# Three of four MLP GEMMs as seven block products, and each MLP over all tokens in turn

## The reference

```python
def _attn_ref(q, k, v, tau):                     # q, k, v: 1 x 6016 x 256
    qn = q / (np.linalg.norm(q, axis=1, keepdims=True) + 1e-06)
    kn = k / (np.linalg.norm(k, axis=1, keepdims=True) + 1e-06)
    s = kn.transpose(0, 2, 1) @ qn / tau         # 256 x 256
    s = s - s.max(-1, keepdims=True)
    a = np.exp(s)
    a /= a.sum(-1, keepdims=True) + 1e-09
    return v @ a

x = _attn_ref(q, k, v, tau).reshape(6016, 256)
h = x @ moe_w_in                                 # 256 x 2048
x = (h * np.cos(h)) @ moe_w_out                  # 2048 x 256
h = x @ moe2_w_in
y = (h * (1.0 / (1.0 + np.exp(-h)))) @ moe2_w_out
```

## Time and profile before

| | us |
|---|---|
| median of 3 executions (1125.02 to 1125.83) | 1125.22 |
| the profiled execution, span from first to last instruction | 1123.1 |
| PE busy in it | 1108.1 |
| ACT busy | 578.9 |
| DVE busy | 551.9 |
| POOL busy | 0.8 |
| first fold matmul starts | 60.07 |
| last matmul starts | 1119.57 |

### The profile page before, as it was taken

The page is one execution under the profiler, slowest core; times in us unless marked ns, Lnnn a source line. Parts: engine busy times, 40 slices in busy tenths (PEclk is TensorE's granted clock), DMA queues, the critical chain, the costliest instruction groups (busy, mean ns, idle before and its releaser), DMA issues.

```text
span 1123.1 us, 12484 instructions
## 1 busy us (share of the span) xinstructions
PE 1108.1 (99%) x4952; PEld 917.3 (82%) x4952; DVE 551.9 (49%) x505; ACT 578.9 (52%) x604; POOL 0.8 (0%) x7
## 2 busy tenths in 40 slices
PE   7999999999999999999999999999999999999998
PEld 7978788888888888888888888888888888889888
DVE  8879852562462463364265255256246346326312
ACT  7777753554554454355455455355455445446443
POOL 0000000000000000000000000000000000000000
PEclk9989999999999999999999999999999999999999
DMA  8823000000000000000000000000000000000000
GB/s 286 285 95 96 36 1 19 20 1 19 19 0 19 0 19 19 0 19 0 19 19 0 19 19 0 19 19 0 19 19 0 14 0 19 0 1 20 1 19 15
DMA packets 15539, 33.31 MB, mean 30 GB/s; under 512 B 1184, under 2 KB 5792, under 8 KB 15520
## 3 DMA queue, kind: packets, MB, share of 16 engines
q1 hardware_dynamic: 15520, 33.03, 8.7%
HBM read 26.87 MB, written 6.16 MB: 29 GB/s over the span
## 4 chain that ended last, share of the span: by engine, by line
PE 98%; DVE 1%; DMA 0%; ACT 0%; issue 0%; DVEq 0%
PE h_ps L638 16%; PE h_ps L639 16%; PE h_ps L637 16%; PE x_ps L637 8%; PE x_ps L638 8%; PE x_ps L639 8%; PE y_ps L638 8%; PE y_ps L637 8%; PE y_ps L639 8%; PE x_ps L652 2%; PE h_ps L654 1%; PE h_ps L656 1%; DMA qk_raw<-qk 0%; DVE qk_lo L457 0%; DVE work L510 0%; DVE work L517 0%
## 5 line engine op out<-in xcount | busy, mean ns | idle before, releaser
L498 DVE TENSOR_TENSOR g_lo<-work,g_hi 128x1024 fp32r<-128x1024 f32 (+1 forms) x192 | 230.4, 1200 | 285.1 <-ACT g_hi L378 273.0
L510 DVE SCALAR_TENSOR_TENSOR work<-work,h_ps 128x1024 f32<-128x1024 int32 (+1 forms) x96 | 115.1, 1199 | 156.4 <-ACT work L361 156.3
L361 ACT ACTIVATE work<-h_ps 128x1024 int32<-128x1024 f32 (+1 forms) x96 | 96.9, 1010 | 167.3 <-PE h_ps L639 167.2
L378 ACT ACTIVATE g_hi<-h_ps 128x1024 fp32r<-128x1024 f32 (+1 forms) x96 | 96.8, 1008 | 160.0 <-PE y_ps L639 124.7
L376 ACT ACTIVATE work<-h_ps 128x1024 f32<-128x1024 f32 (+1 forms) x96 | 96.8, 1008 | 135.8 <-PE h_ps L639 135.8
L637 PE MATMUL x_ps<-g_hi,w1out_hi 128*128 128x512 f32 (+1 forms) x384 | 150.0, 391 | 0.4 <-DVE x_lo L484 0.4
L638 PE MATMUL h_ps<-v_lo,wu_hi 128*128 128x512 f32 (+1 forms) x384 | 149.8, 390 | 0.0
L639 PE MATMUL h_ps<-v_hi,wu_lo 128*128 128x512 f32 (+1 forms) x384 | 149.8, 390 | 0.0
L638 PE MATMUL x_ps<-g_lo,w1out_hi 128*128 128x512 f32 (+1 forms) x384 | 149.8, 390 | 0.0
L637 PE MATMUL h_ps<-v_hi,wu_hi 128*128 128x512 f32 (+1 forms) x384 | 149.5, 389 | 0.0
L639 PE MATMUL x_ps<-g_hi,w1out_lo 128*128 128x512 f32 (+1 forms) x384 | 149.2, 389 | 0.0
(11 more groups left out here) (111 smaller groups left out, 1151.4 us busy)
## 6 DMA issues: line engine op xcount, KB each, us to landing
qk_raw<-qk SPq DMA_DIRECT2D x23, 512.0 KB, 4.7
v_raw<-vT SPq DMA_DIRECT2D x11, 512.0 KB, 3.8
yT<-y_out SPq DMA_DIRECT2D x11, 512.0 KB, 2.8
w_raw<-w_in SPq DMA_DIRECT2D x8, 512.0 KB, 5.4
w_raw<-w_out SPq DMA_DIRECT2D x8, 512.0 KB, 4.0
v_raw<-vT SPq DMA_DIRECT2D x1, 384.0 KB, 3.3
yT<-y_out SPq DMA_DIRECT2D x2, 192.0 KB, 1.9
qk_raw<-qk SPq DMA_DIRECT2D x1, 256.0 KB, 4.6
```

Source lines behind the costliest of these rows:

```text
L361: nc.scalar.activation(work_int[:, slot, :, 0:n], h, ACT.Identity, bias=0.25).then_inc(turns_ready, 1)
L378: nc.scalar.activation(g_hi[:, slot, :, 0:n], h, ACT.Silu).then_inc(g_hi_ready, 1)
L498: nc.vector.tensor_tensor(g_lo[:, slot, :, 0:n], work[:, slot, :, 0:n], g_hi[:, slot, :, 0:n], ALU.subtract).then_inc(g_ready, 1)
L510: nc.vector.scalar_tensor_tensor(out=work[:, slot, :, 0:n], in0=work_int[:, slot, :, 0:n], scalar=0.25, in1=h, op0=ALU.subtract, op1=ALU.s ...
```

## The change

Each step now takes a 2 x 2 block matrix of weights (two halves of the depth by two pairs of hidden blocks) with a 2 x 2 block of activations (two halves of the depth by two halves of a tile's tokens). In place of eight block products it forms seven, with sums and differences of the blocks as operands (the Winograd form of Strassen's scheme): `hidden(i, q)` is product i of step q. This is done for the first GEMM of both MLPs and the second of MLP 2. The second GEMM of MLP 1 stays as it is, in eight groups (`output1`).

- **Tiles.** Twelve tiles of 500 or 504 tokens, in two halves of 250 or 252, so that all MLP matmuls have 250 or 252 columns in place of 512. A tile has four steps of four hidden blocks.
- **Order.** MLP 1 runs over all tiles (steps 0 to 47), then MLP 2 (steps 48 to 95). x is stored to DRAM by tile and loaded again as MLP 2's input. All loops over steps are unrolled.
- **PSUM.** Products 1, 6, 7 and 4 accumulate one after the other in the same bank (two banks alternate by step), and ACT copies the sum out behind 1, 6 and 7 (`s1`, `s2`, `s3` into `s_part`). DVE adds products 2, 5 and 3 from banks 2 and 3 to these copies (`c11`, `c22`, `c12` into `h`). The fourth block stays in its bank.
- **Forms.** The activations' eight forms are made per tile from a DMA-loaded tile: three POOL ops of sums, ACT rounding all seven used ones (`hi_of_form`), POOL the rests (`lo_of_form`). For MLP 2's second GEMM DVE makes forms of g each step (`t13`, `t2`, `t4`), and DVE combines the seven products once per tile (`combine`), behind ACT copies of four of them.
- **Weights.** MLP 1's folded weights get their forms by DVE (pieces 0 and 1) and POOL (2 and 3) at the start. MLP 2's weights get theirs during MLP 1's tiles 2 to 9 by POOL and ACT, go to DRAM, and are loaded at the turn between the MLPs into the space of MLP 1's.
- **Precision and passes** are unchanged; the attention stage is too, but for where its PSUM tiles lie.

The diff is cut to the products, the forms, and the orders of the loops. `in1(q)` and `in2(q)` tell whether step q lies in MLP 1 or 2, M1 is 48, STEPS 4 and LAST 98.

```diff
+PRODUCTS = {1: (1, 1), 2: (3, 3), 3: (7, 2), 4: (2, 7), 5: (4, 4), 6: (6, 6), 7: (5, 5)}
...
+    x_scr = [nc.dram_tensor(f"x_scr{t}", [P, 4, HALF], F32, kind="Internal").ap() for t in range(TILES)]
+    w_scr = [nc.dram_tensor(f"w_scr{k}", [P, 2, 7, 2, P], F32, kind="Internal").ap() for k in range(2 * STEPS)]
...
+                def load_form(t):
+                    n = N[t % TILES]
+                    if t > 0:
+                        sp.wait_ge(xf_ready, t)
+                    if t < TILES:
+                        src = v_of[t]
+                    else:
+                        sp.wait_ge(x_stored, 16 * (t - TILES + 1))
+                        src = x_scr[t - TILES][:, :, 0:n]
+                    sp.dma_start(form[:, 0:4, 0:n], src).then_inc(form_landed, 16)
+
+                def store_x(t):
+                    sp.wait_ge(x_moved, 2 * (t + 1))
+                    sp.dma_start(x_scr[t][:, :, 0:N[t]], xo[:, :, 0:N[t]]).then_inc(x_stored, 16)
+
...
+                def sums_of_form(t):
+                    n = N[t % TILES]
+                    pool.wait_ge(form_landed, 16 * (t + 1))
+                    nc.gpsimd.tensor_tensor(form[:, 4:6, 0:n], form[:, 0:1, 0:n].broadcast_to([P, 2, n]),
+                                            form[:, 1:3, 0:n], ALU.subtract).then_inc(form_sum, 1)
+                    pool.wait_ge(form_sum, 3 * t + 1)
+                    nc.gpsimd.tensor_tensor(form[:, 6, 0:n], form[:, 2, 0:n], form[:, 4, 0:n],
+                                            ALU.subtract).then_inc(form_sum, 1)
+                    pool.wait_ge(form_sum, 3 * t + 2)
+                    nc.gpsimd.tensor_tensor(form[:, 7, 0:n], form[:, 3, 0:n], form[:, 6, 0:n],
+                                            ALU.subtract).then_inc(form_sum, 1)
+
+                def lo_of_form(t):
+                    n = N[t % TILES]
+                    pool.wait_ge(xf_hi_ready, t + 1)
+                    nc.gpsimd.tensor_tensor(xf_lo[:, t % 2, :, 0:n], form[:, 1:8, 0:n], xf_hi[:, t % 2, :, 0:n],
+                                            ALU.subtract).then_inc(xf_ready, 1)
...
+                for t in range(1, 2 * TILES):
+                    if t + 1 < 2 * TILES:
+                        sums_of_form(t + 1)
+                    if 2 <= t < 2 + 2 * STEPS:
+                        sums_of_raw(t - 2)
+                    if t + 1 < 2 * TILES:
+                        lo_of_form(t + 1)
+                    if 2 <= t < 2 + 2 * STEPS:
+                        lo_of_raw(t - 2)
...
+                def s1(q):
+                    n = width(q)
+                    act.wait_ge(p_done[1], q + 1)
+                    if q >= 1:
+                        act.wait_ge(c11_ready, q)
+                    nc.scalar.activation(s_part[:, 0, :, 0:n], banks[:, q % 2, :, 0:n], ACT.Copy).then_inc(s1_ready, 1)
...
+                for q in range(LAST + 1):
+                    if live(q):
+                        s1(q)
+                    if q == M1 + 2:
+                        move_x(TILES - 1)
+                    if in1(q - 1):
+                        turns(q - 1)
+                    if in2(q - 1):
+                        silu(q - 1)
+                    if live(q):
+                        s2(q)
+                    if in1(q - 2):
+                        hi_of_g(q - 2)
+                    if in2(q - 1):
+                        hi_s(q - 1)
+                    if live(q):
+                        s3(q)
+                    if in1(q - 1):
+                        sine(q - 1)
+                    if in2(q - 1):
+                        hi_13(q - 1)
+                    if in1(q):
+                        turns21(q)
+                    if in2(q):
+                        silu21(q)
+                    if in2(q - 1):
...
+                    if s == 2 and t + 1 < 2 * TILES:
+                        hi_of_form(t + 1)
+                    if s == 3 and 2 <= t < 2 + 2 * STEPS:
+                        hi_of_raw(t - 2)
+                    if s == 2 and 1 <= t < TILES:
+                        move_x(t - 1)
+                    if s == 1 and TILES + 1 <= t:
+                        copy_out(t - TILES - 1)
...
+                def c11(q):
+                    n = width(q)
+                    dve.wait_ge(p_done[2], q + 1)
+                    dve.wait_ge(s1_ready, q + 1)
+                    if in1(q - 2):
+                        dve.wait_ge(g_ready, q - 1)
+                    if in2(q - 2):
+                        dve.wait_ge(sil_ready, q - 2 - M1 + 1)
+                    nc.vector.tensor_tensor(h[:, q % 2, 1, :, 0:n], banks[:, 2, :, 0:n], s_part[:, 0, :, 0:n],
+                                            ALU.add).then_inc(c11_ready, 1)
...
+                for q in range(LAST + 1):
+                    if live(q - 1):
+                        c12(q - 1)
+                    if in1(q - 2):
+                        gate(q - 2)
+                    if in1(q - 1):
+                        phase21(q - 1)
+                    if live(q):
+                        c11(q)
+                    t, s = q // STEPS, q % STEPS
+                    if s == 2 and TILES + 1 <= t:
+                        combine(t - TILES - 1)
+                    if in2(q - 2):
+                        lo_24(q - 2)
+                    if in1(q - 1):
+                        phase(q - 1)
+                    if in1(q - 2):
+                        lo_of_g(q - 2, 0, lo_odd_ready)
+                    if in1(q - 2) and in2(q - 1):
+                        lo_of_g(q - 2, 1, lo_even_ready)
+                    if in2(q - 1):
+                        t13(q - 1)
+                        t2(q - 1)
+                        t4(q - 1)
+                        lo_s(q - 1)
+                    if live(q):
+                        c22(q)
+                    if in1(q - 2) and not in2(q - 1):
+                        lo_of_g(q - 2, 1, lo_even_ready)
+                    if in1(q - 1):
+                        gate21(q - 1)
+                    if in2(q - 1):
+                        lo_13(q - 1)
+                    if q == 0:
+                        move_fold(3)
 
             @block.tensor
...
-                def hidden(ph, p):
-                    mlp, tile, s0, before, before_tile = ph
-                    n = width(tile)
-                    if p == 0:
-                        if mlp == A:
-                            pe.wait_ge(v_ready, tile + 1)
-                        else:
-                            pe.wait_ge(x_ready, tile + 1)
...
+                def hidden(i, q):
+                    n, s, t = width(q), q % STEPS, q // STEPS
+                    w, x = PRODUCTS[i]
+                    wt = h1w[s] if in1(q) else h2w[s]
+                    to = {1: q % 2, 6: q % 2, 7: q % 2, 4: q % 2, 2: 2, 5: 3, 3: 3}[i]
+                    if i == 1:
+                        if s == 0:
+                            pe.wait_ge(xf_ready, t + 1)
+                        if q < STEPS:
+                            pe.wait_ge(h1w_ready[s], 1)
+                        if M1 <= q < M1 + STEPS:
+                            pe.wait_ge(h2w_landed[s], 16)
+                        if in1(q - 2):
+                            pe.wait_ge(g21_ready, q - 1)
+                        if in2(q - 2):
+                            pe.wait_ge(sil21_ready, q - 2 - M1 + 1)
+                    if i == 2 and q >= 1:
+                        pe.wait_ge(c11_ready, q)
+                    if i == 6:
+                        if q < STEPS:
+                            pe.wait_ge(h1w_ready[s], 2)
+                        pe.wait_ge(s1_ready, q + 1)
+                    if i == 7:
+                        pe.wait_ge(s2_ready, q + 1)
+                    if i == 4:
+                        pe.wait_ge(s3_ready, q + 1)
+                    if i == 5 and q >= 1:
+                        pe.wait_ge(c12_ready, q)
+                    if i == 3:
+                        pe.wait_ge(c22_ready, q + 1)
...
+                        mm = three_passes(banks[:, to, j, 0:n], wt[:, 0, w - 1, j, :], wt[:, 1, w - 1, j, :],
+                                          xf_hi[:, t % 2, x - 1, 0:n], xf_lo[:, t % 2, x - 1, 0:n],
+                                          i in (1, 2, 5) and j == 0, True)
+                    mm.then_inc(p_done[i], 1)
...
+                for q in range(LAST):
+                    if in1(q):
+                        if in1(q - 1):
+                            hidden(3, q - 1)
+                        hidden(1, q)
+                        if in1(q - 3):
+                            output1(q - 3, (0,))
+                        hidden(2, q)
+                        hidden(6, q)
+                        hidden(5, q)
+                        if in1(q - 3):
+                            output1(q - 3, (1, 2))
+                        hidden(7, q)
+                        if in1(q - 3):
+                            output1(q - 3, (3, 4, 5))
+                        hidden(4, q)
+                        if in1(q - 3):
```

(17 more changed lines are left out.)

1014 lines of the change are left out of this document (640 added, 374 removed).

## The result

| | before | after |
|---|---|---|
| median, us (4 runs each) | 1125.53 | 1189.77 |
| range of the runs | 1125.02 to 1126.10 | 1188.62 to 1190.75 |
| profiled span | 1123.1 | 1187.6 |

What follows compares the result with a forecast made beforehand. TensorE, busy 99%, was taken as the bound, its time proportional to columns. Terms 60.1 + 5.1 + 8.3 + 956.3 + 15 + 36 + 3 + 4 + 4.5 gave a span of 1092.3 us, hence 1094 us; range 1066 to 1150.

Steps and rivals of the forecast that it cites:

- after the last matmul's start: Kernel's end: last adds and a 512 KB store after the last matmul, 4.5 us where before has 3.5.
- the term for the tile boundaries: Each tile's end: late ScalarE copies and output combination cost 1 us a tile in MLP 1, 2 in MLP 2; 36 us.
- its sign for this: VectorE in the MLPs: operations of 1500 elements would last 1.7 us even beside POOL.
- POOL stands in VectorE's way: Rival, MLP tiles: POOL's operations hold off VectorE's with two SBUF inputs; 77 us in place of 36, 1135 us; chance 0.36.
- The matmul term: MLP matmuls: 8352 of about 250 columns at 114.5 ns each, priced by columns; 956.3 us.
- The third rival: MLP matmuls: those under 256 columns cost more, 117 ns each; 21 us more, 1115 us; chance 0.12.
- The start: Folds and steps 0 to 2: fold 2 starts 5.7 us late, then ring waits; 15 us, between 10 and 22.
- The turn: Between the MLPs: first output product waits for x_moved, two copies and a late ScalarE; 3 us.
- cheap boundaries: Rival, tile boundaries: they cost next to nothing, 12 us instead of 36, and 12 at the start; 1067 us; chance 0.15.
- the column count: The MLP GEMMs go from 2.310 million to 2.094 million columns, 9.4% fewer.
- the room on VectorE and ScalarE: MLP 1 step: VectorE needs 8.5 us and ScalarE 6.7 against TensorE's 10.3, so TensorE stays the bound.
- x through DRAM: MLP tiles: a 512 KB store and a load per tile, 2.8 and 3.8 us, covered by matmuls, costed at nothing.

Runs made afterwards that it cites:

- the run of halves: The kernel before with each MLP and fold matmul issued as two of half the columns (512 as two of 256, 384 as two of 192); 1147.3 us (1.0196).
- The filled version: The version of 1119.7 us with 145 matmuls whose result nobody reads, in front of twelve products where TensorE waits; 1114.0 us (0.9901).
- the version of 1119.7 us: Changed kernel, GpSimd's loop work moved to VectorE, start and turn rearranged, form rounding split, first product copied before fold 1's forms; 1119.7 us (0.9947).
- the stream of quarters: The kernel before with each matmul of 512 columns issued as four of 128 (384 as four of 96); 4039.3 us (3.59).

## Why the prediction was wrong, step by step

The table sets the terms of my sum against the changed kernel. A term "above an even stream" (the start behind fold 2's wait, the boundaries, the turn) adds, over a stretch, what each distance of starts of 132 ns or more has above 116.9, the mean of the others.

| term | forecast | after |
|---|---|---|
| head, cold and other folds | 73.5 | 76.3 |
| 8352 matmuls | 956.3 | 976.3 |
| start, fold 2's wait and up to 150 us | 15 | 34.8 |
| boundaries: MLP 1 from 150 to 600 us | 12 | 33.2 |
| turn, 600 to 700 us | 3 | 19.3 |
| boundaries: MLP 2 and tail | 28 | 41.9 |
| after the last matmul's start | 4.5 | 6.0 |
| sum | 1092.3 | 1187.5 |

In the first row the first fold starts 1.0 us later, at 61.1, and the folds take 15.2 us in place of 13.4, as some twenty of them run at the lower clock and not twelve. (The stretches don't end at tile borders, so the split of the middle rows is rough: 600 to 700 us holds some boundaries too.)

**The rival was the case.** The step that failed is the term for the tile boundaries: its 36 us put what GpSimd's operations do to VectorE at nothing, and its sign for this, operations of 1500 elements that last 1.7 us even beside GpSimd, came out as 5.10 us. "POOL stands in VectorE's way" had the mechanism. I had priced the operation of 1750 elements at 4.1 us and it takes 3.98; I had put the cost at 77 - 36 = 41 us, and moving the work to VectorE gave back 40. That the sizes agree so well is partly luck. The rival had 48 us in MLP 1 and, with the tail, 33 in MLP 2, where the table has 33.2 and 41.9; and moving the work took 30 us from MLP 1 (33.2 to 3.3) but only 11 from MLP 2 (41.9 to 31.1), so most of what MLP 2 loses stays with GpSimd idle. TensorE's waits there, after 700 us, are mostly for ScalarE's first copy (13.7 us) and for c22 (11.4).

With no row showing the two engines together I gave the rival 0.36 against 0.37 for the forecast, and the bounds of 1.6 to 5.4 us for one operation reached from no effect to 1177; the measured 1189.8 lies beyond even that, as the terms below failed too. The Trainium skill (SBUF — State Buffer, section Who interferes with whom) says that a VectorE instruction with two SBUF inputs contends with a GpSimd instruction that reads SBUF, that the ports they share are an exclusive lock, and that the order of issue decides who blocks. The trace agrees for two-operand operations on GpSimd (the multiply behind one takes 5.10 us where 1.71 is due, and one behind the multiply is stretched in turn); with one operand the hold-off was 0.8 us of 2.8 at most, less than a lock would give. The Trainium skill (GPSIMD Engine Reference, section Elementwise — side-by-side cycle accounting) led to an estimate of 3.8 us for the operation of 1750; the trace has 3.98. Had I taken the exclusion as the base case, the forecast would have been 1135: the right sign, and still 55 us short.

**The matmul term was mis-sized, by 20 us.** I drew a line through 512, 384 and 256 columns and went on along it to 250, at 114.5 ns. (The 172.4 ns at 384 columns came from a count that takes in matmuls cut by the window; their starts are 174.5 ns apart. The line gives 114.5 at 250 all the same.) The third rival, 117 ns, was right: 116.6 to 117.0. In the run of halves 256 columns came to 116.3. That costs 8352 x 2.4 ns. Of the 79 us by which even 1114 us lies above what the columns alone promised (1125.2 - 89.8 = 1035.4), it makes 20.

**The start was mis-sized, by 20 us.** Fold 2 started 8.0 us late, where I had 5.7, and the first step began at 81.63, not near 78. Then the ring had the waits that I had named, of 2.4 to 4.9 us, but the sum knew no lower clock after 65.15 us. 169 MLP matmuls of the changed kernel start at the lower clock, 213 ns apart where 117 are due, some 16 us in all: 73 of them before 140 us, 64 between 636 and 736 us, and 16 each at 1033 and at 1176 us. The filled version shows that this hangs on the waits: a wait at the start is paid again in the clock.

**The turn was mis-sized, by 16 us**, some of which belongs to the boundaries. I had looked at x_moved alone (3 us). TensorE's waits between 600 and 700 us:

```profile
PE banks L1032 <- ACT xo L577: 4.1, 1, 4.1
PE banks L1032 <- DVE work L834: 2.7, 1, 2.7
PE banks L1032 <- ACT s_part L534: 2.4, 2, 1.9
PE banks L1032 <- DVE h L799: 2.4, 2, 1.6
...
```

That on x_moved is the first, 4.1 us; the others come to 8.6 us together, nearly three times my term, and the clock fell behind them at 636.8, 660.7 and 677.8 us.

**The boundaries**, 40 us forecast with the tail, came to 75, against the rival's 81. With GpSimd's work on VectorE those of MLP 1 are 3.3 us in 450, so the "cheap boundaries" case was right there; those of MLP 2 fell from about 3.5 to 2.6 us a tile, and came to 1.2 in the version of 1119.7 us.

**What held**: the column count, the room on VectorE and ScalarE (the nine VectorE operations of a step of MLP 1 fit as soon as they last what they last alone), the DMAs, which show in none of TensorE's waits, and x through DRAM, at no cost that shows.

**Open**: whether the 111 to 117 ns are the weight load's alone. Halves of 192 columns are 5 ns faster than those of 256, so the columns still count a little at the full clock. At the lower one 96, 128 and 250 columns cost the same, 213 ns. And why the stream of quarters never left the lower clock is open too.

## What to carry to other kernels

Work given to an idle GpSimd is not free when VectorE runs on two SBUF operands: here VectorE did it in half the time, and both engines' work together took VectorE no longer (1006.9 us) than its own had taken beside GpSimd (1013.2). A scheme that trades wide matmuls for more and narrower ones should be priced from a stretch of nearly that width; the run that halves the matmuls of the kernel before, at 116.3 ns for 256 columns, had most of it. And where TensorE waits often, count its lower clock behind the waits as a cost of its own.
